# Weights times x by Strassen's algorithm in a two-layer feed-forward after attention: seven products of halves for eight

## The reference

```python
q_bits = (np.einsum('bhsd,dk->bhsk', q, proj) > 0)   # k likewise; 6 bits make a bucket
mask = q_bucket[:, :, :, None] == k_bucket[:, :, None, :]
scores = np.where(mask, scale * q @ k.T, -1e9)        # 2 batches, 8 heads, 768 x 768, head size 64
x = softmax(scores) @ v                               # laid out as 1536 tokens x 512

h = x @ w_in                                          # 1536 x 512 @ 512 x 2048
x = np.where(h > 0, h, np.exp(np.minimum(h, 0)) - 1) @ w_out      # 2048 x 512

h = x @ w_in2
out = (s * np.maximum(h, 0) ** 2 + b) @ w_out2
```

## Time and profile before

| | us |
|---|---|
| median of three runs | 755.49 |
| lowest, highest | 755.17, 756.86 |
| the profiled execution | 755.06 |
| its span, first to last instruction | 753.3 |
| busy in the span: TensorE | 745.9 |
| VectorE | 397.5 |
| ScalarE | 315.8 |
| GpSimd | 313.5 |

### The profile page before, as it was taken

One profiled execution on the slowest core, in us unless ns is written; L12 is line 12 of the kernel. 1 busy time (PEld: TensorE's weight loads), 2 busy tenths in 40 slices (PEclk: granted clock), 3 DMA queues, 4 the chain that ended last, 5 costly groups with the idle time before them and its releaser, 6 DMA issues.

```text
span 753.3 us, 11777 instructions
## 1 busy us (share of the span) xinstructions
PE 745.9 (99%) x3762; PEld 641.3 (85%) x3762; DVE 397.5 (53%) x757; ACT 315.8 (42%) x614; POOL 313.5 (42%) x252
## 2 busy tenths in 40 slices
PE   8999999999999999999999999999999999999997
PEld 5999999999998888888888888888888888888886
DVE  6888888888877765333334333443234323243233
ACT  7888888888873122222123212231222212121211
POOL 6898989988999992000001666720000000000000
PEclk9999999999999999999999999999999999999999
DMA  5775575465533342000000232300001000010001
GB/s 167 177 173 132 127 177 145 115 154 136 133 89 93 113 131 67 0 1 1 0 1 0 84 111 84 110 2 1 0 1 56 0 0 0 0 56 0 0 0 56
DMA packets 44466, 50.67 MB, mean 67 GB/s; under 512 B 8260, under 2 KB 33172, under 8 KB 44436
## 3 DMA queue, kind: packets, MB, share of 16 engines
q1 hardware_dynamic: 44148, 50.02, 24.6%
q10 hardware_dynamic: 288, 0.26, 0.1%
HBM read 29.45 MB, written 3.19 MB: 43 GB/s over the span
## 4 chain that ended last, share of the span: by engine, by line
PE 97%; ACT 1%; DMA 1%; POOL 0%; DVE 0%; issue 0%; SPq 0%; DVEq 0%; POOLq 0%
PE h_ps L681 35%; PE acc L703 35%; PE pt_ps L646 8%; PE pv_ps L661 4%; PE pv_ps L662 4%; PE s_ps L633 4%; PE s_ps L632 4%; DMA raw<-qk_dram 1%; PE prep_ps L614 1%; PE prep_ps L613 1%; PE prep_ps L615 1%; ACT kt L798 0%; ACT qqk L798 0%; POOL qqk L447 0%; DVE pt_lo L917 0%
## 5 line engine op out<-in xcount | busy, mean ns | idle before, releaser
L876 ACT ACTIVATE r_sb<-h_ps 128x512 f32<-128x512 f32 x96 | 57.4, 598 | 361.6 <-PE h_ps L681 361.6
L681 PE MATMUL h_ps<-xt_hi,wb_hi 128*128 (+1 forms) x288 | 112.1, 389 | 0.0
L681 PE MATMUL h_ps<-xt_lo,wb_hi 128*128 (+1 forms) x288 | 112.0, 389 | 0.0
L681 PE MATMUL h_ps<-xt_hi,wb_lo 128*128 (+1 forms) x288 | 112.0, 389 | 0.0
L1008 DVE TENSOR_SCALAR g_sb<-e_sb,sb_scale 128x512 f32<-128x512 f32 x48 | 27.7, 578 | 158.3 <-ACT e_sb L879 158.3
L910 DVE TENSOR_SCALAR_CACHE_REDUCE probs<-s_ps 128x768 f32<-128x768 f32 x96 | 91.9, 958 | 10.2 <-PE s_ps L633 7.4
L1006 DVE SCALAR_TENSOR_TENSOR g_sb<-e_sb,h_ps 128x512 f32<-128x512 f32 x48 | 33.0, 687 | 117.3 <-ACT e_sb L879 116.7
L804 ACT ACTIVATE probs<-probs,row_min 128x768 f32<-128x768 f32 x96 | 90.0, 938 | 2.0 <-DVE probs L910 1.1
L646 PE MATMUL pt_ps<-ident_sb,probs 128*128 128x128 f32 x576 | 80.1, 274 | 1.7 <-DVE pt_lo L917 1.7
L1014 DVE TENSOR_TENSOR g_lo<-g_sb,g_hi 128x512 fp32r<-128x512 f32 x96 | 77.1, 803 | 3.3
L646 PEld LDWEIGHTS pt_ps<-ident_sb,probs 128*128 128x128 f32 x576 | 68.2, 141 | 8.1 <-issue 2.7
(11 more groups left out here) (95 smaller groups left out, 1531.5 us busy)
## 6 DMA issues: line engine op xcount, KB each, us to landing
w_raw<-w_in_dram SPq DMA_DIRECT2D x32, 256.0 KB, 2.8
w_raw<-w_out_dram SPq DMA_DIRECT2D x32, 256.0 KB, 2.9
raw<-qk_dram SPq DMA_DIRECT2D x15, 384.0 KB, 5.7
qqk<-kt SPq DMA_DIRECT2D x15, 384.0 KB, 4.1
...
```

Of the source, the lines that this page charges most:

```text
L681: last = mm(bank[:], w[a][:, kt * P:(kt + 1) * P], x[b], start=n == 0, stop=n == 3 * KT - 1)
```

## The change

The product h = w_in^T x is computed for two blocks of hidden units and one chunk at a time, a step; there are 8 steps a chunk (`STEPS`) and 48 in all. Weights and x are each cut into 2 x 2 quarters: the weights by k halves (256 of 512 rows) and by the two blocks, x by k halves and by token halves (256 of 512). In Winograd's form of Strassen's algorithm four sums of quarters of each side (S1 to S4, T1 to T4) and three quarters as they are enter seven products; seven additions make the four quarters of h.

A product is two k-tiles and three matmuls of 256 columns, into the first half of one of the four banks, and VectorE adds products to sums as they come (`sums`). ScalarE copies the first product to SBUF (`p1_sb`). h now lies in SBUF (`h_sb`), the gate is made in place, and its rounding has moved from VectorE to ScalarE.

The weights in are loaded anew for each step, 2 x 256 KB, also in chunks 2 and 3; VectorE forms their sums (`combine_w`), ScalarE rounds all seven parts (`round_w`), GpSimd subtracts for the seven low parts (`weights`), two steps, one step and one step ahead. The weights out are loaded apart and still split once a layer, by GpSimd (`weights_out`): two steps' worth in attention, the others in steps 0 to 5, those of layer 2 in steps 18 to 25. x stays in fp32 (`x32`); for each chunk its four sums are made by VectorE in steps p = 2 and 3 of the chunk before, rounded by ScalarE and subtracted by GpSimd in p = 3 to 6. For the first chunk and the first step GpSimd does all of this within attention (`first_parts`), in place of the split of x and of four weight slots. TensorE's order is hidden(step), output(step - 1). All loops over steps are written out instead of looping.

```diff
-EARLY = 4
-HBANKS, GRING, SRING = 4, 3, 3
+STEPS = DF // (2 * P)
+LAYER = CHUNKS * STEPS
+EARLY = 2
+HBANKS, GRING, SRING = 4, 4, 3
+S1, S2, S3, S4, A11, A12, A22 = range(7)
+T1, T2, T3, T4, B11, B21, B22 = range(7)
+Q = CHUNK // 2
+DK = KT // 2
+PRODUCTS = ((A11, B11, 0), (S2, T2, 1), (S1, T1, 2), (S3, T3, 3), (A12, B21, 0), (S4, B22, 1), (A22, T4, 3))
+U2, U4, U3, C22, C11, C12, C21 = range(1, 8)
...
 # GpSimd, in attention
+            def first_parts(i, half):
+                if (i, half) == (1, 0):
+                    combine_w0(S1, S3)
...
+                elif (i, half) == (3, 0):
+                    split_sums(0).then_inc(w0_split, 1)
+                elif (i, half) == (3, 1):
+                    weights_out(0, 0)
+                elif (i, half) == (4, 0):
+                    weights_out(0, 1)
...
+                elif (i, half) == (6, 1):
+                    pool.wait_ge(x0_hi, 3)
+                    split_x(0, B11)
...
                 if prev:
                     sum_x(i - 1, 0)
-                    split_x(i - 1, 0)
+                    scale_x(i - 1, 0)
+                    first_parts(i, 0)
...
 # GpSimd, after attention
+            weights(1)
+            for n in range(2):
+                sum_x(PAIRS - 1, n)
+                scale_x(PAIRS - 1, n)
+            for step in range(2 * LAYER):
+                q, p = step // STEPS, step % STEPS
+                if 2 <= step + 1 < 2 * LAYER:
+                    weights(step + 1)
...
+                if EARLY <= step + EARLY < STEPS:
+                    weights_out(0, step + EARLY)
+                elif 0 <= step - (LAYER - STEPS + 2) < STEPS:
+                    weights_out(1, step - (LAYER - STEPS + 2))
+                if q + 1 < 2 * CHUNKS and 3 <= p < 7:
+                    n = p - 3
+                    pool.wait_ge(xb_hi_done, 4 * q + n + 1)
+                    split_x(q + 1, (B11, B22, T1, T3)[n]).then_inc(xb_split, 1)
...
 # TensorE
+            def hidden(step, part=range(NP)):
...
+                    if n == 0:
...
+                        wait(pe, w_split, step)
...
+                        wait(pe, added, SUMS * (step - 1) + C11)
...
+                    elif n == 4:
+                        pe.wait_ge(p1_kept, step + 1)
+                    elif n == 5:
+                        pe.wait_ge(added, SUMS * step + U2)
+                    else:
+                        pe.wait_ge(added, SUMS * step + U3)
...
+                    for k in range(DK):
+                        for m, (i, j) in enumerate(((0, 0), (0, 1), (1, 0))):
+                            last = mm(h_ps[bank][:, 0:Q], w[i][:, k * P:(k + 1) * P], x[j][:, k * Q:(k + 1) * Q],
+                                      start=k == 0 and m == 0, stop=k == DK - 1 and m == 2)
+                    last.then_inc(product_done, 1)
...
-                if not more and k == HIDDEN_UNIT:
-                    hidden(0, 0, 0, range(1))
...
             times_v(PAIRS, -2, range(4, TILES))
-            hidden(0, 0, 1)
+            hidden(0, range(4))
             times_v(PAIRS, -1, range(TILES))
...
+            hidden(0, range(4, NP))
+            for step in range(1, 2 * LAYER):
+                hidden(step)
+                output(step - 1)
+            output(2 * LAYER - 1)
...
 # ScalarE
+            round_w(1)
+            for step in range(2 * LAYER):
...
+                copy(p1_sb[step % 2][:], h_ps[0][:, 0:Q]).then_inc(p1_kept, 1)
+                if 2 <= step + 1 < 2 * LAYER:
+                    round_w(step + 1)
+                for f in range(2):
...
+                    nc.scalar.activation(r_sb[f][:], h_sb[f][:], ACT.Relu, scale=1.0 if layer else -1.0).then_inc(r_done, 1)
...
+                for f in range(2):
+                    act.wait_ge(g_made, 2 * step + f + 1)
+                    wait(act, g_free, 2 * step + f + 1 - GRING)
+                    copy(g_hi[(2 * step + f) % GRING][:], h_sb[f][:]).then_inc(g_hi_done, 1)
...
+                if q + 1 < 2 * CHUNKS and 3 <= p < 7:
+                    n = p - 3
+                    act.wait_ge(xb_combined, 4 * q + 4 if n == 3 else 4 * q + 3)
+                    round_x(q + 1, (B11, B22, T1, T3)[n])
...
 # VectorE
+            for step in range(2 * LAYER):
+                q, p = step // STEPS, step % STEPS
+                if step:
+                    sums(step, (U2, U4, U3, C22, C11, C12, C21))
+                gate(step)
+                if step + 2 < 2 * LAYER:
+                    combine_w(step + 2)
+                if q + 1 < 2 * CHUNKS and 2 <= p < 4:
+                    combine_x(q + 1, p == 3)
+                if p == 0 and q > CHUNKS:
+                    keep_out(q - CHUNKS - 1)
```

More of the change, by code:

```diff
@@ L507, in pair @@
+            def pair(i):
+                prev, nxt, place = i > 0, i < PAIRS - 1, i
                 split_third(i, 0)
@@ L729, in unit @@
                 transpose_probs(i, u, k, 1)
-                if not more and k == HIDDEN_UNIT:
-                    hidden(0, 0, 0, range(1, KT))
                 if third == 0 and not (first and k < 2 * HT):
@@ L1034, in x_cols @@
+            keep_out(CHUNKS - 1)
 def x_cols(i, n):
```

581 lines of the change are left out of this document (376 added, 205 removed).

## The result

The changed kernel takes 810.95 us (median of four runs, 808.67 to 812.72) beside 755.34 for the kernel before on the same chip: a ratio of 1.073, 95% interval 1.0696 to 1.0763. It is 55.6 us slower; 792 was predicted, within a range of 747 to 815; of the narrower 772 to 812 that the prediction gave its own case, the result is at the very top.

A forecast was written before the change was run, and what follows sets the result against it. TensorE's matmul slots were taken to bound the kernel. 755.1 - 19.2 (slots) + 29 (weights out) + 20 (x) + 1.4 (output copies) + 5 (attention's end) + 1 (attention) = 792.3; predicted 792 us, range 747 to 815.

The forecast's parts named there:

- slots, 48 steps: TensorE's feed-forward steps: 256-column slots of 0.120 us take a step from 10.88 to 10.48, saving 19.2 us.
- weights out and x, steps 2 to 6 and 19 to 26: Steps with GpSimd's extra splits: 2.1 us a step for weights out, 4.0 a chunk for preparing x.
- x in the other three chunks: Preparing the next x block in p = 2 to 6: 4.0 us a chunk, 20 us over all five chunks.
- attention's end to step 2: Between attention and the first steps: waits for transposes, step 1's weights, sums and step 2's split, 5 us.
- attention: GpSimd's added work in the head pairs: pairs 3 and 4 late, most absorbed, 1 us, bounds 0 and 4.
- The shared resource: VectorE and GpSimd exclude each other for whole instructions, alternating; eight VectorE instructions a step are of the excluded kind.
- The late engine and the wait: In the steps TensorE would wait on VectorE's sums, not on GpSimd's split of the weights.
- Weights-out steps: Steps 0 to 5 and 18 to 25: 12.6 us each, 2.1 over 10.48, 29 us for fourteen.
- The clock: TensorE's clock falling to 1.2 GHz in fourteen stalled steps, +147 us; part of a rival above 815, chance 0.10.
- The rival of hidden collisions: VectorE and GpSimd collisions in the steps stay hidden and TensorE still sets the pace: 747 us, chance 0.20.
- half-seen ones: VectorE waits once a step for one GpSimd instruction, slack takes the rest: 768.7 us, chance 0.17.
- Slots paced by the weight load: Products with the weights in paced by weight loads of 0.188 us: +118 us; part of a rival above 815, chance 0.10.

The follow-up runs named there:

- e8_before_256: The kernel before, its products with the weights in computed as 48 matmuls of 256 columns in place of 24 of 512: 771.65 us.
- e2_few: The changed kernel, most GpSimd subtractions and casts from step 2 on cut to 8 columns, VectorE and ScalarE work whole: 754.05 us.
- e1_no_wo: The changed kernel without GpSimd's split of weights out in the steps and its loads; blocks split in attention are reused: 777.85 us.
- e4_order: e3_load_early, with GpSimd waiting with weights out and low parts of x until VectorE's combinations of weights are done: 777.94 us.
- e3_load_early: The changed kernel, with the load of the second block of weights out near the head of pair 4's transfers, not their middle: 807.37 us.
- e5_fill: The changed kernel, with 6 to 18 zero-tile matmuls in each of nine steps where TensorE would wait: 812.26 us.

## Why the prediction came out as it did

The sum, 792.3, was 18.7 us short of 811. Measured by its own terms, from the lengths of steps:

| term | predicted | measured |
|---|---|---|
| slots, 48 steps | 10.48 us a step, -19.2 | 10.50, -18.2 |
| weights out and x, steps 2 to 6 and 19 to 26 | 13 x 2.1 + 2 x 4.0 = 35.3 | 18.8 + 26.6 = 45.4 |
| x in the other three chunks | 12.0 | 5.6 + 4.0 + 3.0 = 12.6 |
| layer 2's output copies | 1.4 | 2.3 |
| attention's end to step 2 | 5 + one step with weights out, 2.1 = 7.1 | 8.6 |
| attention | 1 | 6.7 |

Attention's end is the 26.2 us from the first product to step 2, less 17.6 of slots. Attention is the first product's start, 231.7, against the same place in the kernel before without its first twelve slots, 224.6, less the 0.5 for the last transposes that the prediction had counted in the row above. The measured terms add to 57.4 us; the two profiled executions lie 57.0 apart.

- **Slots:** right. The 0.120 us of the tail's six matmuls held for 2016; e8_before_256 shows the 13 ns by themselves. An estimate from the figures of the Trainium skill ("TensorE: Matmul & The Clock Gate", Back-to-back issue gap), 48 x 109 against 24 x 216 ns a step, has that kernel lose 2 us; it lost 16, and the measurement decides.
- **The shared resource:** right, and it is the cause. e2_few takes away columns of GpSimd alone and 57 us with them; the sums from PSUM stay at 0.41 to 0.43 in all kernels. The rule of the Trainium skill ("SBUF — State Buffer", Who interferes with whom) of a lock held for a whole instruction is what the earlier trace rows and the step at 309 show; a shared bandwidth would not give 2.56 and then 0.41.
- **The late engine and the wait:** right: VectorE's first sum, 36.8 of 43.6 us of waits in the steps.
- **Weights-out steps:** right in kind and nearly in size, 29 against 33.1 by e1_no_wo. Where they stand alone the steps are 11.30 (2), 11.63 (24) and 12.53 (25 and 26), where 12.6 was said for each.
- **What was too small in the sum, first:** the two extra works were priced apart and added. Where they meet, GpSimd's 4.4 + 3.4 + 2.4 and VectorE's 4.4 excluded us are more than a step, and the lateness is handed on: step 6 takes 17.48 us where 2.1 + 1.5 over 10.48 would be 14.1. VectorE's own subtractions for x count too. They were priced at next to nothing because a plain step has slack, but weights out have used the slack up: step 3, with no x work of GpSimd's in it, takes 15.85 where 12.6 was said. Together this is 10 of the missing 19. e4_order, with the same work in another order, still has its longest steps where the two meet.
- **Second:** in attention I counted GpSimd's instructions but not what they wait for. A load that lands 4.3 us late stops an engine that is busy 24.4 of 26.5 us, and all of it comes through. e3_load_early shows 3.6 (by the medians) to 4.7 (by the first product's start) of the 5.7 missing us.
- **Third:** the waits between attention and step 2 add to 5.7 (1.33, 0.85 and 3.51), under the 7.1 that I gave, but with the clock at 0.89 from 228 to 260 the stretch is 8.6 over its slots at full clock. What the clock alone costs there was not tried.
- **The clock:** left at 1.00 in the sum, and "no gap" was the argument; the change made the gaps itself. It fell as the Trainium skill's page "TensorE: Matmul & The Clock Gate" (HAM oscillation) says, to 0.69 in the window 510 to 520, but e5_fill shows that it costs nothing in the nine steps that were filled. That the sum could leave it out was luck: the argument for it was wrong, and only the wait for VectorE made the slow slots free.

The rival of hidden collisions was out by 64 us and that of half-seen ones by 42. Slots paced by the weight load are excluded by e8_before_256, and a clock that costs time in the steps by e5_fill.
